# Two unused pads ahead of the weight cells and ahead of the T operands of a windowed-attention and two-FFN kernel

## What is computed

```python
keep = is_sink | in_window                       # 4 sinks, a window of 128
a = softmax(where(keep, q @ k.T / 8, -1e9)); x = a @ v
g = x @ w_gate; x = (g * sigmoid(g) * (x @ w_val)) @ w_out      # 512 -> 1536 -> 512
h = x @ w_in;   x = (max(h, 0) + alpha * min(h, 0)) @ w_out2    # 512 -> 2048 -> 512
```

## The kernel before

| tensor | first byte before | remainder of 2,048 | first byte after | remainder |
|---|---|---|---|---|
| raw_weights, part_sum | 1,152, 9,344 | 1,152 | the same | 1,152 |
| w_hi, w_lo | 11,392, 50,304 | 1,152 | 12,288, 51,200 | 0 |
| x_hi, x_lo | 89,216, 109,696 | 1,152 | 90,112, 110,592 | 0 |
| h_hi, h_lo, gate_sb | 130,176, 138,368, 146,560 | 1,152 | 131,072, 139,264, 147,456 | 0 |
| scratch | 155,872 | 224 | 156,800 | 1,152 |
| x2_sb and t4_hi, t4_lo | 184,800, 188,896 | 480 | 186,368, 190,464 | 0 |
| q_sb and t_hi | 192,992 | 480 | 194,560 | 0 |
| k_sb; v_sb | 201,184; 209,632 | 480; 736 | 202,752; 211,200 | 0; 256 |
| t_lo; value_sb | 205,280; 217,568 | 480; 480 | 206,848; 219,136 | 0; 0 |

## Time and profile before

### The profile page before, as it was taken

One profiled execution on the slowest core, in us unless ns is written; L12 is line 12 of the kernel. 1 busy time (PEld: TensorE's weight loads), 2 busy tenths in 40 slices (PEclk: granted clock), 3 DMA queues, 4 the chain that ended last, 5 costly groups with the idle time before them and its releaser, 6 DMA issues.

```text
span 626.9 us, 9436 instructions
## 1 busy us (share of the span) xinstructions
PE 619.8 (99%) x3094; PEld 490.0 (78%) x3094; DVE 403.4 (64%) x691; ACT 245.7 (39%) x596; POOL 454.6 (73%) x598
## 2 busy tenths in 40 slices
PE   8999999999999999999999999999999999999997
PEld 5677777777778888888788888888888888888886
DVE  5954757656585946474746474888777557755474
ACT  5754563653645523031303030544544423442150
POOL 5889888788778999898999483799999987710000
PEclk9999999999999999999999999999999999999999
DMA  9423543411222122020212331101112222000004
GB/s 292 142 67 119 186 136 102 119 36 52 86 82 70 33 68 68 33 68 34 68 37 65 101 101 35 50 3 29 58 65 67 69 67 89 14 0 1 1 18 184
DMA packets 29007, 45.67 MB, mean 73 GB/s; under 512 B 2880, under 2 KB 8768, under 8 KB 28960
## 3 DMA queue, kind: packets, MB, share of 16 engines
q1 hardware_dynamic: 28672, 44.81, 23.0%
q10 hardware_dynamic: 288, 0.26, 0.2%
HBM read 41.92 MB, written 3.15 MB: 72 GB/s over the span
## 4 chain that ended last, share of the span: by engine, by line
PE 97%; ACT 2%; DVE 1%; issue 0%; POOL 0%; DVEq 0%; ACTq 0%; POOLq 0%
PE ffn_ps L2092 29%; PE att_ps L2067 24%; PE ffn_ps L2007 16%; PE att_ps L2092 8%; PE ffn_ps L2067 7%; PE att_ps L1947 4%; PE att_ps L1898 2%; PE att_ps L1918 2%; PE att_ps L2007 1%; PE att_ps L1959 1%; PE att_ps L1892 1%; ACT scratch L2140 1%; PE att_ps L2099 1%; PE ffn_ps L1947 1%; PE att_ps L1894 0%; PE att_ps L1890 0%
## 5 line engine op out<-in xcount | busy, mean ns | idle before, releaser
L1751 POOL TENSOR_TENSOR w_lo<-raw_weights,w_hi 128x512 fp32r<-128x512 f32 (+1 forms) x126 | 155.2, 1232 | 10.1
L1750 POOL CAST w_hi<-raw_weights 128x512 fp32r<-128x512 f32 (+1 forms) x126 | 80.2, 636 | 27.5 <-PE ffn_ps L2092 17.9
L2478 DVE TENSOR_TENSOR scratch<-ffn_ps,scratch 128x512 f32<-128x512 f32 x108 | 73.9, 686 | 35.0 <-PE ffn_ps L2092 34.2
L1779 POOL TENSOR_TENSOR w_lo<-part_sum,w_hi 128x256 fp32r<-128x256 f32 x80 | 60.0, 751 | 6.4
L2007 PE MATMUL ffn_ps<-x_hi,w_hi 128*128 128x512 f32 x152 | 61.6, 405 | 0.0
L2007 PE MATMUL ffn_ps<-x_hi,w_lo 128*128 128x512 f32 x152 | 59.4, 391 | 0.0
L2007 PE MATMUL ffn_ps<-x_lo,w_hi 128*128 128x512 f32 x152 | 58.8, 390 | 0.0
L2092 PE MATMUL ffn_ps<-h_hi,w_hi 128*128 128x512 f32 x130 | 51.6, 397 | 0.0
L1831 POOL TENSOR_TENSOR scratch<-scratch,inv 128x264 f32<-128x264 f32 (+1 forms) x48 | 30.4, 634 | 28.2 <-DVE inv L2349 28.1
L2092 PE MATMUL ffn_ps<-h_hi,w_lo 128*128 128x512 f32 x130 | 50.7, 390 | 0.0
L2092 PE MATMUL ffn_ps<-h_lo,w_hi 128*128 128x512 f32 x130 | 50.7, 390 | 0.0
(11 more groups left out here) (213 smaller groups left out, 1577.5 us busy)
## 6 DMA issues: line engine op xcount, KB each, us to landing
raw_weights<-pieces SPq DMA_DIRECT2D x122, 256.0 KB, 2.7
k_sb<-kt SPq DMA_DIRECT2D x12, 264.0 KB, 3.9
out<-scratch SPq DMA_DIRECT2D x12, 256.0 KB, 2.0
q_sb<-qt SPq DMA_DIRECT2D x11, 256.0 KB, 4.0
v_sb<-vt SPq DMA_DIRECT2D x10, 256.0 KB, 3.1
v_sb<-vt SPq DMA_DIRECT2D x1, 512.0 KB, 6.6
scratch<-vs SPq DMA_DIRECT2D x1, 384.0 KB, 7.5
q_sb<-qt ACTq DMA_DIRECT2D x2, 128.0 KB, 3.0
```

The source lines that it names most:

```text
L1750: chain(pool.tensor_copy(hi, raw[:, r % n_raw, at]))
L1751: last = pool.tensor_tensor(lo, raw[:, r % n_raw, at], hi.bitcast(F32), ALU.subtract)
L1779: pool.tensor_tensor(lo, s, hi.bitcast(F32), ALU.subtract).then_inc(split_done, 1)
L2478: ins = dve.tensor_tensor(to, back_ps(key), total, ALU.add)
```

## The change

Two tensors that nothing reads or writes are declared, one of 224 and one of 160 columns, and `table_out`, of which one column is used, becomes 16 columns wide (64 bytes in place of 32). No instruction is added, removed or moved: on each engine the sequence of instructions, their operands, shapes and waits are the same, and only the addresses differ, as in the table above.

```diff
@@ -1348,6 +1348,8 @@
         raw = sb("raw_weights", [P, n_raw, PIECE])
         part_sum = sb("part_sum", [P, 2, PIECE // 2])
+
+        sb("ahead_of_weights", [P, 224])
         w_hi = sb("w_hi", [P, n_cells, PIECE], F32R)
         w_lo = sb("w_lo", [P, n_cells, PIECE], F32R)
@@ -1361,7 +1363,7 @@
-        table_out = sb("table_out", [P, 1])
+        table_out = sb("table_out", [P, 16])
@@ -1380,6 +1382,7 @@
         pt_sb = scratch[:, late + P_COLS:late + P_COLS + PT_COLS].rearrange("p (r m h n) -> p r m h n", r=2, m=2, h=2)
+        sb("ahead_of_sums", [P, 160])
         with nc.sbuf_tensor("x2_sb", [P, n_k, TB], F32) as x2_sb:
@@ -2127,7 +2130,7 @@
-                act.activation(table_out[:, :], bias[:, (u - 1) % 4, 0:1], ACT.Exp, scale=0.0).then_inc(table_done, 1)
+                act.activation(table_out[:, 0:1], bias[:, (u - 1) % 4, 0:1], ACT.Exp, scale=0.0).then_inc(table_done, 1)
```

## The result

The changed kernel takes 624.16 us (median of 6 runs) beside 628.61 us of the kernel before; the ratio is 0.9929, 95% interval 0.9911 to 0.9947, so 4.4 us faster. Forecast were 623.6 us. The number came out almost as worked out, and the sets of strips show the gain where it was put; the reason given for it did not survive the first four experiments.

What follows compares the result with a forecast made beforehand. The prediction took the interval between successive matmuls on PE to bound the kernel. 628.64 us less 4.6 (T operands) and 0.4 (lingering behind attention), with nothing for the rest, gave 623.6 us, range 602 to 629.2 us.

Steps and rivals of the forecast that it cites:

- What bounds the kernel: On PE: nearly every microsecond is the time in which matmuls follow each other; PE busy 619.8 of 626.9 us.
- Part 1: T operands in the 20 sets of 42 strip matmuls: start remainder 480 to 0 gives 0.23 us per set, 4.6 us.
- 7.2 ns: Extra interval of a matmul whose moving operand is T, read as about 16 columns, 64 bytes.
- Part 2: Attention tensors move to multiples of 64, shortening the 12 feed-forward matmuls behind each burst: 0.4 us, bounds 0 and 1.8.
- the lingering: Matmuls directly after T still pay some 5 ns; those behind an attention burst also run slightly slow.
- Part 3: Weight cells, x and h, remainder 1,152 to 0, no longer crossing a 2 KB boundary: taken as 0, bounds 0 and 31.0 us.
- The 13.3 ns: Time each matmul carries beyond its columns at 2.4 GHz: a cost per matmul or of crossing a 2 KB boundary.
- Part 4: Engines beside PE (ACT, POOL) hardly see the address and stay hidden behind PE: 0 us.
- rival D: Slower: POOL's splits lengthen as source and target differ by 1,152 bytes in phase; 641 us at 25%, chance 0.08.
- Rival C: Nothing changes, 628.6 us: the 7 ns belong to where T lies or to the sets; chance 0.16.
- A: The 64-byte step alone: moving operands not starting at a multiple of 64 bytes cost 7 ns; 623.6 us, chance 0.56.

Runs made afterwards that it cites:

- the first four experiments: e1, e2, e3 and e4, each a different placement of operands in the kernel before: 627.54, 628.75, 628.69 and 637.84 us.
- e3: Kernel before with only a pad of 8 columns (32 bytes) ahead of the weight cells, so everything moves together: 628.69 us, ratio 0.9993.
- f4: Kernel before with pads of 8 columns ahead of the cells and 168 ahead of T, all starting at remainder 1,184 of 2 KB: 624.18 us.
- e2: Kernel before with only the pad of 224 columns ahead of the cells; cells, x, h at multiples of 2 KB, T at remainder 1,376: 628.75 us.
- e8: Changed kernel with the 576 backs of stage C taking only the upper two bytes of each element as bf16, still 4 bytes apart: 623.88 us.
- e9: Changed kernel with the 576 backs of stage C reading one constant tile as packed bf16, both operands from the same start: 619.61 us.
- e4: Kernel before with two pads of 8 columns and table_out widened, so that weight cells alone are 32 bytes off a multiple of 64: 637.84 us.
- e1: Kernel before with only table_out widened to 16 columns, T at remainder 512, cells, x and h at 1,152: 627.54 us, ratio 0.9984.
- g1: Changed kernel with x and h 256 bytes beyond multiples of 2 KB, cells and T as in it: 624.04 us, ratio 0.9920.
- f3: Changed kernel with T1 4, T3 16 and T2 384 bytes beyond a multiple of 512, T4 untouched: 626.82 us, ratio 0.9967.
- e10: e9 with the stationary operand 32 bytes behind the start of the moving one: 619.66 us.

## Why the prediction was right, and its reason wrong

1. *What bounds the kernel.* Right: the interval between matmuls moved the time. Waits moved it too, by 0.4 us the other way, which the prediction had at nothing.

2. *Part 1, T, 4.6 us.* The size and the place were right: each of the 20 sets gave 0.23 us by its intervals, and waits in three sets, 0.63 us in place of 0.22, took back a tenth. The step that failed is the one in which 7.2 ns was read as 16 columns and so as one 64-byte piece more per operand, from "480 = 7 x 64 + 32". The change puts all operands at multiples of 2 KB, and with that it both makes T start at a multiple of 64 and makes T's distance to the cells a multiple of 256; in the kernel before, T was wrong in both. No row of before could part the two: all x, h and cells had one common remainder, so no row had a right start with a wrong distance or the reverse. e3 and f4 parted them, and the distance it is: with 1,848 moving operands 32 bytes off a multiple of 64 the backs stayed at 226.7 ns. The prediction named it in its last sentence as what would overturn it, and noted that for x and h the distance keeps its values while for T it does not. That was the place to give it a chance of its own; it had none.

3. *Part 2, 0.4 us of the lingering.* Mis-sized: 0. Behind a burst 12 matmuls still take 2.75 to 2.77 us. A short wait has the same lingering behind it, as the timeline after the wait at 332.96 us shows, so it does not need an address. The lingering behind T went with T's price; part 1 had counted that share of it rightly, with the sets. Why a slower stretch lingers is not shown.

4. *Part 3, nothing from the 2 KB boundary.* Right: e2 and f4, and 9.52 us for 42 backs before and after. The 13.3 ns are not a matter of placement in any run here; e8 and e9 point to columns that lie 4 bytes apart, with the reservation made there. The prediction's pieces of 64 bytes, from which it made both the 13.3 and the 7.2 ns, are left without support: in f4 every moving operand would need a piece more, and none costs more.

5. *Part 4 and rival D.* Right that POOL, ACT and DVE hardly see the address: 454.6 and 454.4 us, 245.7 and 246.1, 403.4 and 403.5. One group moved by 1% (L1782, L1779 before, a mean of 758 in place of 751 ns).

6. *Rival C and the page's rule.* The rule of 16-byte lines (the Trainium skill, "SBUF — State Buffer", "Door 1: The DMA port swizzle") foresees no change here, since all starts before and after were multiples of 16. The runs show 4.4 us from starts that satisfy it before and after, and 9 us in the other direction in e4.

The forecast with A's 5.0 us and the measured 4.4 us agree for two reasons, then: the price was read from the rows and did not depend on its cause, and the change happened to remove both candidates. The second is luck, and so is part of the closeness: part 2 gave nothing of its 0.4 us, the waits took 0.4 us, and 0.2 us came from pieces that no part had. A reader who had used A to place tensors elsewhere would have been wrong, as e1 shows: its condition met, a quarter of the gain.

What stays open is why the distance matters. It was seen with 4-byte columns at the upper clock level, in about the same amount for 4 bytes (235 ns) as for 32 (233), and not with packed bf16; no run shows it at the lower level. No run tells either whether the moving operand is disturbed by its own stationary operand or by the next one, whose load overlaps it (PEld is busy 489.4 us beside PE's 614.8 of 622.5 us): nearly everywhere both have the same distance. Also e1's T at distance 128 costs somewhat less per set (0.17 us over) than 96 does (0.23), and that was not followed further.

## What to carry to other kernels

In a stream of fp32r matmuls like this one, begin the tensors that are moving operands and those that are stationary operands at the same remainder of 256 bytes; which remainder does not matter. Check it by adding up the declarations, since one tensor of a single column between them is enough to shift it (by 32 bytes here), and read it in the chain of waits as the time of a run over its number of matmuls. And when a change removes two candidate causes at once, its result says nothing on which of them it was: shift everything together by a little (as e3 does, and as f4 does with the distance closed), and the absolute and the relative theory part.

## What the runs showed of the hardware that was not expected

- Distance between moving and stationary start, fp32r, 512 columns: 226.7 ns where it is a multiple of 256 bytes (changed kernel, f4, g1), 233.3 ns at 32 bytes (e4, fronts), 235 ns at 4 bytes (f3), 232 ns at 128 bytes (e1, T2). Packed bf16: 216 ns at 0 and at 32 bytes (e9, e10).
- bf16 columns 4 bytes apart go at 225 ns (e8), side by side in one constant tile at 216 ns (e9).
- After a wait of 60 ns in the stream the next eight intervals are 231 ns in place of 226.7 (changed kernel, 333.25 to 335.10 us).
